# Block inversion in a delta-rule attention kernel: identity terms moved from TensorE to VectorE, a masked copy of N and the weight splits moved to GpSimd

## The reference, cut to what matters

```python
for t in range(S):
    kt, vt, bt = (k_n[:, :, t], v[:, :, t], beta[:, :, t, None])
    y[:, :, t] = np.einsum('bhd,bhde->bhe', q[:, :, t], state)
    v_old = np.einsum('bhde,bhd->bhe', state, kt)
    state = state + bt[:, :, :, None] * np.einsum('bhd,bhe->bhde', kt, vt - v_old)
```

## Time and profile before

| | us |
|---|---|
| median of 3 runs | 1106.98 (1105.72 to 1110.4) |
| the profiled execution, its own time | 1101.72 |
| its span, first to last instruction | 1100.0 |
| PE busy in the span | 1019.6 |
| DVE, ACT, POOL busy in the span | 519.5, 366.4, 311.3 |
| one window in the steady part, from one `ksq` on POOL (223.00) to the next (258.98) | 36.0 |

### The profile page before, as it was taken

One profiled execution on the slowest core, in us unless ns is written; L12 is line 12 of the kernel. 1 busy time (PEld: TensorE's weight loads), 2 busy tenths in 40 slices (PEclk: granted clock), 3 DMA queues, 4 the chain that ended last, 5 costly groups with the idle time before them and its releaser, 6 DMA issues. The chain is left out here.

```text
span 1100.0 us, 30946 instructions
## 1 busy us (share of the span) xinstructions
PE 1019.6 (93%) x13260; PEld 889.7 (81%) x13260; DVE 519.5 (47%) x1134; ACT 366.4 (33%) x731; POOL 311.3 (28%) x202
## 2 busy tenths in 40 slices
PE   4898998999999999849999999998699999999998
PEld 3787887888888888738999999997488888888888
DVE  5566666677666665425444444433342423233221
ACT  1455545455555555412222222221221222122111
POOL 3333242334233423015452555524400001000000
PEclk9999999999999999959999999999699999999999
DMA  9312112121212111045343445223201010100000
GB/s 304 122 34 65 55 41 73 55 72 41 72 56 72 41 45 34 16 172 177 100 149 134 172 172 172 79 86 122 65 22 44 15 44 16 48 18 18 19 11 29
DMA packets 58055, 84.90 MB, mean 77 GB/s; under 512 B 28880, under 2 KB 52816, under 8 KB 55376
## 3 DMA queue, kind: packets, MB, share of 16 engines
q1 hardware_dynamic: 52272, 46.94, 13.5%
q0 software_dynamic: 5664, 36.18, 9.7%
HBM read 61.67 MB, written 21.43 MB: 76 GB/s over the span
## 5 line engine op out<-in xcount | busy, mean ns | idle before, releaser
L1081 PE MATMUL hb<-early,last_h 128*128 128x512 f32 x648 | 207.8, 402 | 1.2 <-DVE early L1213 1.2
L1081 PEld LDWEIGHTS hb<-early,last_h 128*128 128x128 f32 x648 | 121.5, 190 | 29.3 <-DVE early L1213 1.6
L1081 PE MATMUL hb<-early,last_l 128*128 128x512 f32 x324 | 129.1, 399 | 0.0
L1219 DVE TENSOR_TENSOR m<-hb,m 128x512 f32<-128x512 f32 x36 | 24.9, 692 | 132.0 <-PE hb L1081 132.0
L329 PEld LDWEIGHTS bank<-t,n_hi 64*64 64x64 f16 x2688 | 65.2, 110 | 24.7 <-issue 8.9
L541 DVE TENSOR_TENSOR p<-bank,cf 128x512 f16<-128x512 f32 x96 | 66.0, 688 | 30.2 <-PE bank L329 29.2
L329 PE MATMUL bank<-t,n_hi 64*64 64x64 f16 x2688 | 72.2, 195 | 6.0 <-issue 5.2
L1081 PE MATMUL ob<-wo_h,early 128*128 128x384 f32 x288 | 75.1, 339 | 0.0
L1081 PEld LDWEIGHTS hb<-early,last_l 128*128 128x128 f32 x324 | 61.6, 190 | 15.0
L1003 POOL TENSOR_TENSOR late<-w_raw,late 128x3072 fp32r<-128x3072 f32 x8 | 54.5, 6811 | 57.7 <-DVE late L943 57.4
L912 ACT CAST ht_h<-ht_bank 128x512 fp32r<-128x512 f32 x56 | 32.9, 587 | 109.3 <-PE ht_bank L866 55.4
(11 more groups left out here) (163 smaller groups left out, 2213.7 us busy)
## 6 DMA issues: line engine op xcount, KB each, us to landing
w_raw<-w POOLq DMA_DIRECT2D x14, 1536.0 KB, 7.4
kq_t<-qh SPq DMA_DIRECT2D x24, 256.0 KB, 3.3
y_sorted<-y_sb SPq DMA_DIRECT2D x31, 192.0 KB, 1.9
x_in<-x_sorted SPq DMA_DIRECT2D x29, 192.0 KB, 2.9
k_raw<-kt_in SPq DMA_DIRECT2D x24, 192.0 KB, 3.2
v_in<-vh SPq DMA_DIRECT2D x24, 192.0 KB, 3.3
k_own<-kh SPq DMA_DIRECT2D x24, 192.0 KB, 3.1
out<-o_sb SPq DMA_DIRECT2D x24, 192.0 KB, 1.8
```

Source lines behind the costliest of these rows:

```text
L1081: ins = pe.matmul(out, a[x], b[y], start=first and i == 0, stop=last and i == 2, skip_group_check=True)
L1219: dve.tensor_tensor(m1[f % 2][:], h_bank[f % 2][1][:, :], m0[f % 2][:], ALU.max).then_inc(m1_out, 1)
```

## The change

- `jacobi`: PE no longer adds the identity; DVE adds it in its eviction instead of masking (`CF_EYE`). The mask to 4x4 blocks is applied once to N, by POOL, in a new tensor `n_base`, and PE multiplies by that. The first `jacobi` waits for `n_base_ready`, no longer for `n_hi_ready`; the first `prod` waits for `n_hi_ready`.
- `resid`: PE no longer adds the identity; DVE evicts with 2I added (`CF_TWO`), where ACT only copied. `inv`: PE no longer adds the transpose of T, since (2I - T + NT) holds that term already.
- The split of the first expert's weights goes from DVE to POOL, in four instructions a window as before.
- `counted` is kept by POOL, just ahead of its `send`, where DVE kept it at the end of `slot`.
- The tables: `kn` and `mask` one slot later, part 9 of `NORM` one slot earlier, the pieces in slots 3, 8, 14, 15.

```diff
-    PRE = {-5: ["kn"], -4: ["mask"]}
+    PRE = {-4: ["kn"], -3: ["mask"]}
-    NORM = {1: [0], 2: [1], 3: [2], 4: [10], 5: [3], 6: [4], 7: [5], 8: [6], 9: [7, 8], 10: [9], 12: [11], 14: [12]}
+    NORM = {1: [0], 2: [1], 3: [2, 10], 5: [3], 6: [4], 7: [5], 8: [6, 13], 9: [7, 8, 9], 14: [11], 15: [12]}
...
             elif what == "jacobi":
                 if lv == 0:
                     pe.wait_ge(gram_out[st], 2 * k + 2)
-                    pe.wait_ge(n_hi_ready[st], k + 1)
+                    pe.wait_ge(n_base_ready[st], k + 1)
                 else:
                     pe.wait_ge(jacobi_out[st], 3 * k + lv)
                 pe.sem_inc(passed_pe, 1)
-                diagonal(ident16, ident_rep, pb, True)
-                each_head(n, eye if lv == 0 else t, pb).then_inc(jacobi_done[st], 1)
+                each_head(nb, eye if lv == 0 else t, pb, first=True).then_inc(jacobi_done[st], 1)
...
-                diagonal(ident16, ident_rep, pb, True)
-                diagonal(neg16, flat(t16[st]), pb, False)
+                diagonal(neg16, flat(t16[st]), pb, True)
                 each_head(n, t, pb)
                 each_head(nl, t, pb).then_inc(resid_done[st], 1)
             elif what == "inv":
                 pe.wait_ge(tt_out[st], (LVS + 1) * (k + 1))
-                pe.sem_inc(passed_pe, 1)
-                each_head(t, eye, ttb, first=True)
                 pe.wait_ge(resid_out[st], k + 1)
                 pe.sem_inc(passed_pe, 1)
-                each_head(pr, tt, ttb).then_inc(inv_done[st], 1)
+                each_head(pr, tt, ttb, first=True).then_inc(inv_done[st], 1)
...
             elif what == "rank":
                 pe.wait_ge(chosen_ready[st], k + 1)
-                if 2 * k + st >= 1:
-                    pe.wait_ge(counted_ready, 2 * k + st)
+                pe.wait_ge(counted_ready, 2 * k + st + 1)
...
-                dve.tensor_tensor(t16[st][:], pb, mask_of(None), ALU.mult).then_inc(jacobi_out[st], 1)
+                dve.tensor_tensor(t16[st][:], pb, of_heads(CF_EYE), ALU.add).then_inc(jacobi_out[st], 1)
+            elif what == "resid":
+                dve.wait_ge(resid_done[st], k + 1)
+                dve.tensor_tensor(p16[st][:], pb, of_heads(CF_TWO), ALU.add).then_inc(resid_out[st], 1)
...
-                dve.tensor_tensor(counted[:], counted[:], chosen[:, to, :], ALU.add).then_inc(counted_ready, 1)
...
+            elif what == "split":
+                pool.wait_ge(gram_out[st], 2 * k + 2)
+                pool.tensor_tensor(n_base[st][:], n_kb_a[par][st][:, :, 0, :], of_heads(CF_BASE), ALU.mult).then_inc(n_base_ready[st], 1)
...
+                pool.wait_ge(counted_ready, to + 1)
+                pool.tensor_tensor(counted[:], counted[:], chosen[:, to, :], ALU.add).then_inc(counted_ready, 1)
```

80 lines of the change are left out of this document (42 added, 38 removed).

## The result

The changed kernel takes 1140.78 us (median of 4 runs, 1136.28 to 1145.55) against 1106.95 for the kernel before in the same comparison. The ratio is 1.0305, 95% interval 1.026 to 1.035: slower by 34 us, where I forecast 25 us faster with a range that ended at 1094. The profiled execution took 1145.55 us.

What follows compares the result with a forecast made beforehand. PE's own instruction stream was taken to bound the attention. Terms 21.8 + 6.7 + 3.5 - 2.4 - 0.3 gave 29.3 us off, less 4 for new waits 25: median 1082 us, 8-in-10 range 1070 to 1094.

Steps and rivals of the forecast that it cites:

- The clock: Attention: the clock falling there was named as a sign of being wrong, with no term in the sum.
- The waits that come with a thinner stream: Attention's 24 stream steps: places that just met would now wait, 4 us back, bounded by nothing and 16.6 us.
- The pairs, 21.8 us: `jacobi` and `resid`: 96 pairs of 64x512 identity matmuls leave PE, 21.8 us off including 0.7 in the first window.
- `inv` by DVE's identity, 6.7, and `resid`: `inv` loses 24 groups of 16 matmuls, 6.7 us off; `resid` loses one pair per stream step, counted among the 96.
- The wait ahead of stream 1's first `jacobi`, 3.5: PE's 4.5 us wait there goes because POOL's `n_base` is ready earlier; 3.5 us taken off.
- `turn`, 2.4 back: PE's `turn` waits 0.2 us for `resid`'s eviction, now on DVE, 12 times: 2.4 us back.
- POOL's queue: POOL reaches `n_base` in time: free at 265.4, needed at 271.6, 6 us of slack, so added work costs nothing.
- Theory B: Set up for the experiments: POOL is the new bound, with `n_base` or what stands behind it late.
- my slower rival: POOL late for stream 0's `n_base`, PE waiting on it: 1122 us, or 1100 if only in split windows; chance 0.04.
- The splits, worth nothing: Moving the weight split off DVE: nothing in the sum, at most the 2.4 us of `turn` waits.
- The tail, 0.3 back: At the attention's end POOL counts instead of DVE, slower and with one more hop: 0.3 us back, once.
- The first window: First window of the attention: matmul pairs 0.40 us apart, so its four pairs add 0.7 us to the gain.

Runs made afterwards that it cites:

- after: The changed kernel itself, all parts of the change, against the kernel before; 1140.78 us, ratio 1.0305.
- thin_before: The kernel before without the four pairs of 64x512 identity matmuls in `jacobi` and `resid`; 1100.51 us, ratio to before 0.9952.
- resid_back: The changed kernel with the `resid` and `inv` identities on PE again and ACT evicting `resid`; 1133.77 us, ratio to before 1.0246.
- moves_only: The changed kernel with the identity part undone, keeping splits and counts on POOL and moved table slots; 1110.96 us, ratio to before 1.0035.
- splits_back: The changed kernel with the weight splits back on DVE in their old slots; 1161.84 us, ratio to before 1.0481.
- score_wide_half: The changed kernel with `score` reading PSUM and 48 useless wide pairs ahead of the first `jacobi` and `inv` waits; 1127.97 us, ratio to before 1.0209.
- before_gaps: The kernel before with 80 always-met waits ahead of stream 0's `rank` matmuls in each step; 1169.11 us, ratio to before 1.0587.
- score_light: The changed kernel with DVE's `score` reading the logits from PSUM instead of SBUF; 1136.4 us, ratio to before 1.0297.

## Why the prediction was wrong

The prices of the matmuls were not the step that failed. The sum failed in two terms: it had none for the clock inside the attention, and it put the waits that come with a thinner stream at 4 us. Together they close the account of the profiled execution: 29.3 us forecast off, 25.5 us more in gaps over 0.9 us (36.5 less 11.0), and 47.8 us more lost to the clock (1143.8 x 0.061 less 1100.0 x 0.020) make +44.0; the spans differ by 43.8. (That the two agree so well is in part luck: the clock's term counts a stretch at the lower level as half lost, also where PE stands in it, and gaps outside 60 to 440 us aren't counted.) Over all runs the clock takes 36.5 us, and at full clock after is 1.1 us below before.

- *The clock (failed, the largest).* "I am wrong if [...] the clock falls inside the attention" was among the signs, but neither the sum nor a rival had a term for it. The earlier trace rows had it in sight: 0.77 at 440 to 500 us, "a stretch at the lower level while PE waits in the tail". I read 1.00 at 60 to 440 us as a property of the stage; it was one of a stream without long gaps.
- *The waits that come with a thinner stream (mis-sized).* "At 0.17 us for each stream step it is 4 us", bounded at 16.6 by evictions laid bare. Measured 25.5. The bound looked at DVE and ACT alone; 13.8 of it are late instruction blocks (24.8 less 11.0), for which the kernel before had 9 stops in its trace and I had no row shown. The other 11.7 are mainly the `rank` waits (9.3), for which neither the sum nor its bound had a term.
- *The pairs, 21.8 us.* Alone (thin_before) they gave 12.7 at full clock and 5.9 in time. The distance of a matmul is worth its price only if the next one is there.
- *`inv` by DVE's identity, 6.7, and `resid`.* Their matmuls (6.7 and 24 pairs at 0.22, 5.3) less 2.4 for `turn` make 9.6; resid_back against after gave 8.7 at full clock. Right, and then lost to the clock.
- *The wait ahead of stream 1's first `jacobi`, 3.5.* It went, as forecast.
- *`turn`, 2.4 back.* In place: `jacobi`'s `t16` makes PE wait 4.1 us in 8 waits, before 2.4 in 8. The timeline above has one of 0.52.
- *POOL's queue.* Right. `n_base` took 1.27 us where I had 1.15, and POOL was idle ahead of it, waiting for DVE: the group of 24 on the page is

```profile
L679 POOL TENSOR_TENSOR n_base<-n_kb_a,cf 128x512 f16<-128x512 f32 x24 | 30.5, 1272 | 266.8 <-DVE n_kb_a L533 266.8
```

  and one step of stream 0, to be held against the earlier trace rows, has the eviction's end at 253.33 (251.84 + 1.49), `n_base` at 253.40 and `jacobi` at 254.78:

```profile
251.84 1.49 DVE L533 TENSOR_TENSOR n_kb_a<-bank,beta_mask 128x512 f32<-128x512 f32 x2
...
253.40 1.28 POOL L679 TENSOR_TENSOR n_base<-n_kb_a,cf 128x512 f16<-128x512 f32 x1 [9.31 <-DVE n_kb_a L533]
...
254.78 0.44 PE L334 MATMUL bank<-ch,n_base 64*64 64x64 f16 x16
255.26 0.69 DVE L537 TENSOR_TENSOR t<-bank,cf 128x512 f16<-128x512 f32 x1 [1.07 <-PE bank L334]
...
255.41 0.62 POOL L721 CAST early<-w_raw 128x512 fp32r<-128x512 f32 x1
255.98 0.20 POOL L696 TENSOR_TENSOR counted<-counted,chosen 128x8 f16<-128x8 f16 x1
```

  The cast took 0.62 us (0.47 to 1.15 forecast), `counted` 0.20 (0.3). What I left out is what the queue does to DVE: I counted only who waits for POOL's results, and `score` waited for POOL's reads. The mean in the earlier trace rows held a sign of it, 1246 ns over subtractions of 0.68 and 1.81 us, the longer ones beside `ksq`. Theory B, which was my slower rival, is refuted by these rows, and for the splits and counts by moves_only; the slower outcome came by another way.
- *The splits, worth nothing.* Wrong in the new kernel: splits_back is 1.7% slower than after (1.0481 to 1.0305 of before). I priced the move in the kernel before, where the casts never met POOL. In the new list, with `n_base` in it and `mask` one slot later, they do, and one subtraction stands longer than it did; together this adds 26.6 us to DVE's list ahead of `t16`.
- *The tail, 0.3 back.* PE's last matmul waits 1.01 us for POOL instead of 0.81 for DVE: 0.2.

```profile
526.50 0.19 POOL L696 TENSOR_TENSOR counted<-counted,chosen 128x8 f16<-128x8 f16 x1 [7.20 <-DVE rows_at L582]
...
526.84 0.17 PE L474 MATMUL bank<-counted,ch 128*128 128x8 f16 x1 [1.01 <-POOL counted L696]
```

- *The first window.* PE's first `jacobi` started at 17.03 us, 0.67 behind the pair that started it in before (16.36 in the earlier trace rows), and waited for `n_base`:

```profile
17.03 0.64 PE L334 MATMUL bank<-ch,n_base 64*64 64x64 f16 x16 [2.17 <-POOL n_base L679]
```

The price of the pairs was right: from there to `turn` it is 4.54 us (17.03 to 21.57) where it was 5.80 (16.36 to 22.16), 0.42 for each of three pairs. But `n_base` came later than `n_hi` had, and took back the 0.7 us that I added for the first window.

What stays open: why a block is fetched late. The fetch that ends a stop starts late by itself, nearly empty DMA engines or not. That PE's instruction stream runs further ahead of PE while a wide matmul is at work would explain why pairs of them, ahead of waits, keep blocks in time; this was only argued. Why score_wide_half loses most of the gain with half of the pairs is open for the same reason. before_gaps shows that stretches of 4 us are enough for the clock to fall; that stretches of 1 to 3 us are enough by themselves is read from the order in time in the sixteen traces and was not isolated. What the whole conflict between DVE and POOL costs is open too, since score_light moved it and did not end it.

## What to carry to other kernels

On a stage where PE is above 90% busy with small matmuls, an instruction taken off PE is worth its distance only while PE never stands still; look for stops inside groups and for the clock in each window of the kernel before, and give both a term. A "free" engine's list is not free if a short operation of a neighbour reads SBUF beside it: compare the longest, not the mean, of the short ones, and look at the next operation when one was mended. And work added to PE ahead of a wait can pay: 96 pairs of useless matmuls and one operand moved to PSUM took after from 1.0305 to 0.9955 of before.

## What the runs showed of the hardware

- PE stops of 1 to 4.2 us inside a group of matmuls, at distances that are multiples of 124 to 125 matmuls, ending in after 2.2 to 3.2 us behind the start of an instruction packet of 16 KB. A stop of 1.9 us in before at 138.62 left the clock at 1.00:

```profile
130.00:137.00 7.00, 6.18 (x190) 5.44 (x185) 3.32 (x12) 3.85 (x8) 0.00 (x0) 1.00 0.24 87
137.00:147.00 10.00, 7.93 (x177) 7.13 (x175) 5.92 (x19) 4.70 (x11) 4.21 (x4) 1.00 0.10 30
```

- A fall of the clock can cost more than the stop that it follows: in after 3.0 us of standing still at 261.76 were followed by 10.2 us at the lower level, at most 5.1 us of work.
- A wait that is met already isn't free on PE: 16 in a row idled it for about 0.46 us, 80 for about 3.9 us.
- An 8-column DVE operation of 0.23 us took up to 2.46 us beside POOL in after, and 0.23 again with one input in PSUM (score_light). A DVE cast of 0.42 us took up to 2.58, and a subtraction of 0.68 up to 5.15, beside three POOL operations in a row (splits_back).
- 106 of 107 falls of the clock between 60 and 440 us, in sixteen traces, began during a stop of PE over 0.9 us or within 2.5 us behind it.
